# First expert of the second mixture: the scalar engine copies two of its seven products, and the gate's small steps stand at other products

## The reference, cut to what matters

```python
logits = x @ w_gate                      # 2304 x 8
P = np.exp(logits - logits.max())
for _ in range(8):                       # Sinkhorn rounds
    P /= P.sum(1, keepdims=True) + 1e-09
    P /= P.sum(0, keepdims=True) + 1e-09
    P *= N / E
for e in range(E):
    h = np.maximum(x @ w1[e], 0.0)
    out += P[:, e:e + 1] * (h @ w2[e])
```

## Time and profile before

| | |
|---|---|
| median of three runs | 1057.57 us |
| profiled execution: own time, span | 1057.44 us, 1055.5 us |
| PE busy | 1005.1 us, 95% of the span |
| DVE, POOL, ACT busy | 748.2, 615.1, 583.7 us |
| first expert of the second mixture, from its first product to the next expert's | 240.47 to about 351.4 us |

### The profile page before, as it was taken

The page is one execution under the profiler, slowest core; times in us unless marked ns, Lnnn a source line. Parts: engine busy times, 40 slices in busy tenths (PEclk is TensorE's granted clock), DMA queues, the critical chain, the costliest instruction groups (busy, mean ns, idle before and its releaser), DMA issues.

```text
span 1055.5 us, 25401 instructions
## 1 busy us (share of the span) xinstructions
PE 1005.1 (95%) x8599; PEld 924.3 (88%) x8599; DVE 748.2 (71%) x1994; ACT 583.7 (55%) x1368; POOL 615.1 (58%) x522
## 2 busy tenths in 40 slices
PE   7999979579999999999999999999999999999998
PEld 5888843029999999999999999999999999999998
DVE  7767741426898867876867778778768777877675
ACT  6777710224466746555655566466546564656552
POOL 6445410004487648684966596568747873877443
PEclk9999988658999999999999999999999999999999
DMA  5773267950200220022002200210040012000111
GB/s 184 262 277 112 71 273 265 408 209 2 81 1 2 81 81 2 2 82 81 2 3 83 81 2 2 99 63 1 14 148 5 2 72 91 2 2 20 61 41 61
DMA packets 36904, 87.81 MB, mean 83 GB/s; under 512 B 2976, under 2 KB 2976, under 8 KB 36768
## 3 DMA queue, kind: packets, MB, share of 16 engines
q1 hardware_dynamic: 36768, 86.07, 22.4%
HBM read 81.35 MB, written 4.72 MB: 82 GB/s over the span
## 4 chain that ended last, share of the span: by engine, by line
PE 41%; POOL 27%; issue 22%; DMA 4%; DVE 4%; ACT 1%; POOLq 1%; ACTq 0%; DVEq 0%
POOL s_split L499 19%; PE bank L775 8%; PE bank L777 7%; PE bank L779 7%; POOL t_split L504 4%; PE bank L568 3%; PE bank L578 3%; PE bank L597 3%; DMA late_raw<-slot_w_in 3%; PE bank L725 2%; PE bank L678 2%; PE bank L615 1%; POOL raw L533 1%; POOL raw L535 1%; POOL raw L537 1%
## 5 line engine op out<-in xcount | busy, mean ns | idle before, releaser
L499 POOL TENSOR_TENSOR s_split<-s_sum,s_split 128x512 fp32r<-128x512 f32 x288 | 372.5, 1309 | 342.2 <-ACT s_split L887 337.0
L1241 DVE SCALAR_TENSOR_TENSOR acc<-bank,gate_now,acc 128x256 f32<-128x256 f32 x441 | 228.6, 519 | 146.8 <-PE bank L779 145.8
L887 ACT ACTIVATE s_split<-s_sum 128x512 fp32r<-128x512 f32 x288 | 181.8, 632 | 247.6 <-PE bank L779 137.8
L775 PE MATMUL bank<-t_split,s_split 128*128 128x256 f32 x1008 | 284.2, 282 | 1.3 <-DVE acc L1235 1.1
L777 PE MATMUL bank<-t_split,s_split 128*128 128x256 f32 x1008 | 282.6, 280 | 0.0
L779 PE MATMUL bank<-t_split,s_split 128*128 128x256 f32 x1008 | 282.6, 280 | 0.0
L775 PEld LDWEIGHTS bank<-t_split,s_split 128*128 128x128 f32 x1008 | 189.4, 188 | 5.1 <-issue 3.4
L779 PEld LDWEIGHTS bank<-t_split,s_split 128*128 128x128 f32 x1008 | 192.6, 191 | 0.0
L777 PEld LDWEIGHTS bank<-t_split,s_split 128*128 128x128 f32 x1008 | 189.4, 188 | 0.0
L775 PE MATMUL bank<-t_split,a 128*128 128x256 f32 x576 | 164.1, 285 | 5.8 <-DVE acc L1235 2.5
L777 PE MATMUL bank<-t_split,a 128*128 128x256 f32 x576 | 162.6, 282 | 0.0
(11 more groups left out here) (167 smaller groups left out, 1952.5 us busy)
## 6 DMA issues: line engine op xcount, KB each, us to landing
raw<-big_w_in SPq DMA_DIRECT2D x15, 2048.0 KB, 8.6
early_raw<-slot_w_in SPq DMA_DIRECT2D x12, 1024.0 KB, 10.5
late_raw<-slot_w_in SPq DMA_DIRECT2D x10, 1024.0 KB, 13.5
slot_raw<-slot_w_in SPq DMA_DIRECT2D x7, 1024.0 KB, 5.2
q_ring<-q_tiles SPq DMA_DIRECT2D x18, 256.0 KB, 4.6
k_ring<-k_tiles SPq DMA_DIRECT2D x18, 256.0 KB, 4.9
v_ring<-v_rows SPq DMA_DIRECT2D x18, 256.0 KB, 2.7
out_rows<-acc SPq DMA_DIRECT2D x18, 256.0 KB, 2.0
```

What stands on the lines that cost most here:

```text
L499: pool.tensor_tensor(s_split[:, i, 1, :, :], s_sum[:, i, :, :], s_split[:, i, 0, :, :].bitcast(F32), ALU.subtract)\
L775: pe.matmul(to, left[:, 0, f, :], t_place(parity, k, 0)[:, f, :], start=(f == 0 and k in FRESH), stop=False, skip_group_check=k not in FRESH)
L887: act.activation(s_split[:, i, 0, :, :], s_sum[:, i, :, :], ACT.Copy).then_inc(s_hi_ready, 1)
L1241: done = dve.scalar_tensor_tensor(out=to, in0=got, scalar=gate, in1=to, op0=ALU.mult, op1=ALU.add)
```

## The change

Three things change, all in the first expert (expert 0) of the second mixture.

The additions of A11 and S1, which were copies (or scaled copies, in pairs 7 and 8) from the bank into `acc` on DVE, are done on ACT by a new function `copy_in`, after the first and after the second `relu_halves` of each pair. DVE's `add_product` returns for them at once; the addition of A12 waits for the copy of A11, that of S2 for the copy of S1 (semaphore `copied_in`), and each counts 2 in `added`. So the product S2, which waited for the addition of A11, now waits for that of A12, and S4 for that of S2 in place of S1's.

The gate's steps must stand at products that open a bank afresh and aren't copied by ACT, which leaves A12 (k = 1) and A22 (k = 4). The logits go from (0, 4) to (0, 1), the maximum from (1, 0) to (0, 4), its sharing from (1, 2) to (1, 1), the first sums from (1, 5) to (1, 4), and the rounds as the table says.

```diff
-    ROUND_AT = [(2, 0), (2, 4), (3, 2), (4, 0), (4, 4), (5, 2), (6, 0), (6, 4)]
+    GATES_AT, MAX_AT, SHARE_AT, EXP_AT = (0, 1), (0, 4), (1, 1), (1, 4)
+    ROUND_AT = [(2, 1), (2, 4), (3, 4), (4, 1), (4, 4), (5, 4), (6, 1), (6, 4)]
+    COPIED = (A11, S1)
...
+            def copy_in(p, k):
+                act.wait_ge(product_ready, PRODUCTS * p + k + 1)
+                t, cols = targets(p, k)
+                scale = 1.0 if p < UNSCALED else gates[:, t, 0:1]
+                act.activation(acc[:, t, cols], bank[bank_of(p, k)][:, 0:HD2], ACT.Copy, scale=scale).then_inc(copied_in, 1)
...
                     relu_halves(n1, (parity1 + p1) % 2, 0, before)
+                    if first:
+                        if p >= UNSCALED:
+                            act.wait_ge(gate_vec, 5 + SINKHORN_ROUNDS)
+                        copy_in(p, A11)
...
                     relu_halves(n1, (parity1 + p1) % 2, 1, before)
+                    if first:
+                        copy_in(p, S1)
...
                 if first:
                     gate_step(p, k)
-                if k in (A12, S4, S3) or (k == A11 and not (first and p == 0)):
+                if first and k in COPIED:
+                    return
+                if k in (S4, S3) or (k in (A11, A12) and not first):
                     dve.wait_ge(added, PER_EXPERT * e + PRODUCTS * p + {A11: 0, A12: 1, S4: 4, S3: 5}[k])
+                if first and k in (A12, S2):
+                    dve.wait_ge(copied_in, 2 * p + (A12, S2).index(k) + 1)
...
-                fresh = first and k in (A11, S1, S2, A22)
+                fresh = first and k in (S2, A22)
...
-                done.then_inc(added, 1)
+                done.then_inc(added, 2 if first and k in (A12, S2) else 1)
```

## The result

The changed kernel takes 1069.2 us (median of 4 runs, 1068.28 to 1071.28) beside 1058.11 for the kernel before in the same comparison: a ratio of 1.0112, 95% interval 1.0095 to 1.0129. It is slower, as forecast, but by 11 us and not by 4: 1069.2 lies outside my range of 1058.5 to 1064.3.

The account below looks back on a forecast made before the run. PE, busy 95% of the span, was taken as the bound. Terms -3.65 + 4.7 + 2.8 + 0.1 + 0.3 = +4.25 us on 1057.44 gave 1061.7 us, 0.4% slower; 80% range 1058.5 to 1064.3.

Parts of the forecast that it names:

- the term -3.65: First expert: PE's three waits for DVE's additions (2.15, 1.13, 0.37 us, before products of pairs 5 to 7) go, -3.65 us.
- rival (a): Rounds (4, 1) and (6, 1): POOL's holds don't come back, new waits 1.1 us each, 1056.4 us; chance 0.08.
- The wait at (4, 1): Pair 4: PE waits for S2 until V+8.05 (V: DVE sees product 0 ready), both scalings held by POOL, +4.7 us.
- the one at (6, 1): Pair 6: PE waits for S2 until V+6.24 (V: DVE sees product 0 ready), scalings held by POOL, +2.8 us.
- rival (b): Round (4, 1): DVE's first scaling comes before POOL's L504, wait 2.7 us in place of 4.7, 1059.7 us; chance 0.13.
- No wait stands in pair 2: At (2, 1) g products of 1.93 us stand ahead of S2, so PE was forecast not to wait.
- PE's readiness for S2: Pairs with a round at product 1: PE ready for S2 3.38 us after DVE sees product 0 ready.
- The k = 4 rounds: Rounds (2, 4) to (6, 4) hold up A22's addition, wanted by the next pair's product 0: +0.1 us in all.
- the two late copies: Pairs 7 and 8: two ACT copies of 0.27 us delay the last scaling of `acc`, +0.3 us, between 0 and 0.54.
- the exchange of the logits: Pair 0: 18 logit matmuls moving to k = 1 cost 0 if the clock rises at the same time.
- rival (c): Pair 0: the clock rises later behind the logits, by 3.9 us, half lost: +1.9, 1063.6 us; chance 0.12.

Follow-up runs that it names:

- the kernel with short POOL work: Changed kernel with POOL's weight work of pairs 4 to 7 of the first expert cut down (low parts memsets, sums 8 of 256 columns): 1060.64 us, ratio 1.0033.
- the better version: Against the kernel before: ACT copies in pairs 0 to 6 except at gate steps, first steps at old places, rounds moved: 1057.56 us, ratio 0.9996.
- the kernel with the long fills: Changed kernel with 24 (pair 4) and 20 (pair 6) useless matmuls put into PE's waits before S2: 1072.09 us, ratio 1.0147.

## Why the prediction was wrong, and where it was right

**Right.** The old waits are gone, as the term -3.65 said, and nothing like them is left but 0.41 us at 367.53, in expert 1. As a size the term was low: pair 5 alone gave 2.97 us for its wait of 2.15, so a wait cost more than PE's idle time. The hold by POOL is the mechanism: the kernel with short POOL work brings both scalings to 0.31 us and the waits to 1.14 and 1.50, which also refutes rival (a). The wait at (4, 1) is 4.39 us where I had 4.7, the one at (6, 1) 3.24 where I had 2.8; rival (b) did not come, the first scaling was held for 2.15 us. No wait stands in pair 2. PE's readiness for S2 was put 0.14 us late, since two gate matmuls of a round take 0.28 us but hold up the next product by 0.13 to 0.14 (267.32 to 267.45); that is small beside the waits. The k = 4 rounds and the two late copies cost what was allowed for them: pairs 5, 7 and 8 show -2.97, -0.24 and +0.41, and the kernel with the copies alone is at 1.0016.

**Right in sum, wrong in its course: pair 6.** I let the first scaling be caught by L533 and the second by L535. POOL's pair of instructions ran earlier against DVE's round: the second one caught the first scaling, which ended at 330.31, 0.18 behind it, and the other went free. I had taken the start of POOL's L533 from a pair without a round.

**Wrong: the exchange of the logits.** "So as long as the rise comes at the same time the exchange is 0. I take 0" is the first step that failed. Pair 0 took +3.92 us in the changed kernel and +3.69 in that with short POOL work, 3.6 and 3.4 without the 0.3 for the gate step that moved in, and it goes away (17.28 us) when the first steps go back. I had the mechanism as rival (c), at 0.12, and gave it half its size: I let the rise be late by 3.9 us, and it was late by eight. Against it I put that "PE has no gap there in either order". The trace of before already showed that a PE without a gap can stay at half clock. Its windows ahead of the first wait:
```profile
228.00:230.00 2.00, 2.00 (x24) 0.64 (x16) 0.00 (x0) 0.00 (x0) 0.00 (x0) 0.50 0.00 0
230.00:232.00 2.00, 2.00 (x12) 1.78 (x8) 0.88 (x3) 1.65 (x5) 0.00 (x0) 0.50 0.29 25
```
PE is busy all the time, in part with matmuls of 8 columns and with weights of 128x32, and the clock stays at half. In the changed kernel the row 244 to 246 is of the same kind: PE busy for 2.00 us of 2.00 with the 18 matmuls of 8 columns, clock 0.50, and still 0.50 over 250 to 252. That small matmuls as such keep the clock down does not follow. In the better version, whose code is the same in this stretch, the clock rose among them:
```profile
230.00:231.00 1.00, 1.00 (x12) 1.00 (x8) 0.10 (x1) 0.86 (x3) 0.00 (x0) 0.78 0.00 0
```
The rule that I named beside the term, from the Trainium skill ("TensorE: Matmul & The Clock Gate", Part 1), that the warm-up is a matter of time under load, does not carry the 0 that I hung on it: PE is busy without a gap in both kernels here, and their clocks rose eight microseconds apart. Nor does the trace of before have only "one rise": between 140 and 230 us its clock rose and fell several times.

**Wrong: a wait priced at its own length.** In "PE at V+8.05: +4.7 us" and "PE V+6.24: +2.8 us" I took PE to go on behind the wait as before it. It went on at half clock for about 3 us each time: +1.4 to +1.5 per wait, by the two kernels that filled the waits (-1.44 and -1.43, -1.51 and -1.42). Even the upper end of the range lacked it. I had read only the waits of the first expert, of 2.15 us and less, behind which the first matmul took 0.39 us. Earlier in the same trace stood the case that I needed, a stall of 4.24 us at full clock with half clock behind it:
```profile
156.26 1.50 PE L660 MATMUL bank<-ident,comb 128*128 128x128 f32 x8 [4.24 <-DVE comb L1076]
157.00:158.00 1.00, 1.00 (x7) 1.00 (x6) 0.00 (x0) 0.76 (x2) 0.00 (x0) 0.50 1.02 422
```

The account, in us: old waits -3.65, new ones +7.63, late rise +3.6, half clock behind the waits +2.9, later start +0.7, sum 11.2, with 10.84 by the traces at expert 1 and 11.09 by the medians. That it closes so well is in part luck. Old and new waits cost more than the idle time that stands for them here, on either side of the sum. And the terms are not what each would give back by itself: the 1.44 us of half clock in pair 4 cover a wait of 1.27 in pair 5.

**The loop returns.** The clock accounts for them as well. In the 13 profiles, the five returns with a fall of the clock behind their stall are the five longest, 103.04 to 105.71 us; the others took 100.97 to 101.73, but for the 102.68 of the kernel with the long fills, which has the second stall.

**Open.** Why the clock falls behind a stall of about 2 us in one profile and not in another. Nothing of the edits was found to decide it: the same 2.15 us before product 0 of pair 5 ended at full clock in the kernel before and at half in the one with the two early fills. The edited kernels were profiled once each, so it isn't shown whether their falls at the returns repeat; the twelve timed runs of the better version lie between 1054.25 and 1059.30 us. Nor is it shown what releases the stall at the returns, for which the profile names only "issue", or what, of columns, rows or the work's spacing, kept the clock down behind the early logits.

## What to carry to other kernels

A stall of the busiest engine is to be priced with what it does to that engine's clock: look through the whole trace for stalls of that length and read the clock behind them, and leave room for half rate behind yours. Then ask what stands next: time won behind one wait can turn up as another. Work moved to a place near a rise of the clock is not free of charge because the engine stays busy. When a stretch that you didn't edit grows longer, read its clock before you call it a mystery. And a piece of DVE work put ahead of a short deadline has to be laid beside POOL's instructions one by one, since a 0.3 us operation can take 2.1.

## What the chip showed that I had not expected

- In these 13 profiles, once the clock had come up in the first expert, it fell behind every stall of PE of 2.52 us and more (2.52, 2.75, 3.24, 3.29 and three of 4.39), behind none of 1.70 or less, and in between it did either: it fell behind 2.15, 2.16, 2.08 (twice), 1.87 and 1.73 (a second stall, close behind one of 1.76), and stayed up behind, among others, 2.15, 2.10, 2.06, 2.02, 2.00 and 1.96. The wait's own windows mostly still read 1.00; the fall shows in the first matmul after it, 0.58 against 0.38 us, or up to 1.5 us after PE has started again.
- The clock then stayed at half for about 3.4 us, and for 6.8 in two cases (behind 2.75, and behind 1.76 and 1.73).
- With eighteen matmuls of 8 columns standing behind the first product instead of the fourth, and PE busy throughout, the clock rose about seven microseconds later, counted from that first product.
- Useless matmuls in waits act on it: nine and six ahead of product 0 gave 2.4 us there, fills inside two stalls 1.4 to 1.5 us each inside their pair, of which the next wait took one back. They need no data that is late, only a bank whose columns nobody reads.
- POOL's memset, which reads nothing, did not hold DVE: L1231 ran in 0.31 us while L516 ran from 298.09 to 299.05. The Trainium skill ("SBUF — State Buffer", Who interferes with whom) speaks of a lock between operations with two SBUF inputs and POOL's reads, and that row agrees, as do the three ends 0.16 to 0.18 us behind an instruction of POOL.
- The loop returns: 101.0 to 101.7 us in both originals and their repeats, and up to 105.71 in kernels that were edited only in the first expert, with a fall of the clock each time that it was over 103. Twice a gain in the first expert, 1.4 and 2.4 us, didn't show in the median at all, and the profile had such falls behind it.
